# Reordering the prelude of an mLSTM-and-two-gated-layers kernel: exponents, reciprocals, first weights and gate columns

## The reference

```
m_new  = max(f + m, i);  f_stab = exp(f + m - m_new);  i_stab = exp(i - m_new)
C = f_stab*C + i_stab * v k^T;   n = f_stab*n + i_stab*k
y = sigmoid(o) * (C q) / max(|n q|, 1)
```

```
x1  = silu(rmsnorm(y) @ w_gate) * (rmsnorm(y) @ w_val) @ w_out       (d_ff = 1536)
out = sigmoid(x1 @ w_gate2) * (x1 @ w_val2) @ w_out2
```

## Time and profile before

| | |
|---|---|
| times of the runs | 470.47, 470.62, 474.57 us; median 470.62 us |
| profiled execution | 470.63 us, span 468.8 us |
| mean granted TensorE clock | 0.999 |
| TensorE matmul busy | 457.6 us, 98% |
| VectorE busy | 225.5 us, 48% |
| ScalarE busy | 184.9 us, 39% |
| GpSimd busy | 27.0 us, 6% |

### The profile page before, as it was taken

How to read it: one execution, slowest core, us unless ns; L and a number is a source line. 1 busy time by engine, 2 the same in 40 slices (tenths; PEclk the granted TensorE clock), 3 DMA queues, 4 the chain that set the end, 5 groups by cost and what they waited for, 6 DMA issues and landing times.

```text
span 468.8 us, 7881 instructions
## 1 busy us (share of the span) xinstructions
PE 457.6 (98%) x3064; PEld 377.5 (81%) x3064; DVE 225.5 (48%) x447; ACT 184.9 (39%) x379; POOL 27.0 (6%) x59
## 2 busy tenths in 40 slices
PE   7899899999999999999999999999999999999997
PEld 4588888878888887888888888888888888888885
DVE  5988657776566453645455552222322222322222
ACT  6755545543543432454454552222322222322222
POOL 4311101101010000000000000000000000000000
PEclk9999999999999999999999999999999999999999
DMA  7664035630201300002322200000000000100001
GB/s 211 193 208 127 24 98 174 197 91 15 72 22 38 124 2 0 2 0 95 97 96 95 83 0 0 2 0 1 25 31 1 0 1 0 57 1 0 1 0 57
DMA packets 15757, 26.30 MB, mean 56 GB/s; under 512 B 2248, under 2 KB 10664, under 8 KB 15720
## 3 DMA queue, kind: packets, MB, share of 16 engines
q1 hardware_dynamic: 15496, 25.68, 17.9%
q10 hardware_dynamic: 224, 0.12, 0.1%
HBM read 23.55 MB, written 1.97 MB: 54 GB/s over the span
## 4 chain that ended last, share of the span: by engine, by line
PE 85%; issue 6%; DVE 5%; ACT 1%; POOL 1%; DMA 1%; SPq 0%; DVEq 0%; POOLq 0%; ACTq 0%
PE bank L1346 50%; PE bank L1408 7%; PE bank L1409 6%; PE bank L1410 6%; PE bank L1416 3%; PE bank L1417 3%; PE pair L1286 2%; PE pair L1263 1%; PE bank L1353 1%; PE pair L1300 1%; PE pair L1252 1%; PE bank L1318 1%; DVE gv_split L1012 1%; PE bank L1333 1%; DMA fi_row<-fi_first 1%
## 5 line engine op out<-in xcount | busy, mean ns | idle before, releaser
L1346 PE MATMUL bank<-x_hi,gv_split 128*128 128x512 f32 (+1 forms) x780 | 236.8, 374 | 2.3 <-DVE hid L1028 1.8
L1346 PEld LDWEIGHTS bank<-x_hi,gv_split 128*128 128x128 f32 x780 | 143.1, 188 | 29.1 <-issue 3.3
L1346 PE MATMUL bank<-x_lo,gv_split 128*128 128x512 f32 (+1 forms) x436 | 161.4, 373 | 0.0
L1041 DVE TENSOR_TENSOR hid<-hid,bank 128x512 f32<-128x512 f32 x48 | 33.0, 687 | 132.4 <-PE bank L1346 132.4
L611 ACT ACTIVATE hid_hi<-hid 128x512 fp32r<-128x512 f32 (+1 forms) x78 | 46.6, 598 | 121.4 <-DVE hid L1041 90.5
L1346 PEld LDWEIGHTS bank<-x_lo,gv_split 128*128 128x128 f32 x436 | 82.0, 188 | 14.2
L604 ACT ACTIVATE hid<-bank 128x512 f32<-128x512 f32 (+1 forms) x78 | 43.9, 562 | 118.0 <-PE bank L1346 87.3
L1048 DVE TENSOR_TENSOR hid_lo<-hid,hid_hi 128x512 fp32r<-128x512 f32 (+1 forms) x78 | 51.3, 658 | 42.7 <-ACT hid_hi L611 42.7
L1408 PE MATMUL bank<-hid_hi,wo_split 128*128 128x512 f32 (+1 forms) x154 | 59.7, 388 | 0.0
L1410 PE MATMUL bank<-hid_hi,wo_split 128*128 128x512 f32 (+1 forms) x154 | 57.5, 373 | 0.0
L1409 PE MATMUL bank<-hid_lo,wo_split 128*128 128x512 f32 (+1 forms) x154 | 57.5, 373 | 0.0
(11 more groups left out here) (164 smaller groups left out, 354.9 us busy)
## 6 DMA issues: line engine op xcount, KB each, us to landing
gv_raw<-wgv SPq DMA_DIRECT2D x24, 384.0 KB, 3.1
qk_tile<-qk SPq DMA_DIRECT2D x24, 160.0 KB
wo_raw<-wo SPq DMA_DIRECT2D x24, 160.0 KB, 3.2
v_sb<-v SPq DMA_DIRECT2D x12, 168.0 KB, 4.3
gate<-og SPq DMA_DIRECT2D x12, 160.0 KB, 3.7
k_sb<-k SPq DMA_DIRECT2D x10, 160.0 KB, 4.5
outT<-y_out SPq DMA_DIRECT2D x6, 256.0 KB, 2.0
outT<-y_tail SPq DMA_DIRECT2D x3, 128.0 KB, 2.3
```

The lines of the kernel that those rows point to most:

```text
L1041: ins = nc.vector.tensor_tensor(h, h, v_ps[:, 0:size], ALU.mult)
L1346: mm = pe.matmul(ps[:, 0:size], lhs, rhs, start=(i == 0), stop=whole and i == len(passes) - 1)
```

## The change

All of it lies in the prelude and unit 0.

- TensorE issues all four `early_exponents` ahead of the four `early_outputs`. GpSimd makes the four copies that these need (`select_rows`) ahead of `keep_logs(1)`; copies 2 and 3 wait for exponents 2 and 3.
- The denominators of tiles 0 and 1 lie in one tile and get one `max` and one reciprocal (`first_denominators`), which wait for both `magnitude`s. `first_quotients(0)`, `first_quotients(1)` and `apply_gate(1)` follow.
- The rest of the first weights is made in two halves: the gate half in front of `weight_rows(0)`, the value half behind `rest_x(1)`. `round_gv(0)` on ScalarE moves ahead of `raise_gate` and of both `magnitude`s, `gate_tanh(1)` ahead of `magnitude(0)`.
- `load_gv(0)` is issued ahead of the two `load_gate`.
- `turn_gates(0)` leaves the prelude; it, `turn_gates(1)` and `exponents(2)` now follow `value_products(0)` instead of standing around `gate_products(0)`.

```diff
+            load_gv(0)
             load_gate(0)
             load_gate(1)
-            load_gv(0)
...
-            for i in range(2):
+            for i in range(4):
                 select_rows(i)
             keep_logs(1)
-            for i in range(2, 4):
-                select_rows(i)
...
             gate_tanh(0)
+            round_gv(0)
             raise_gate()
+            gate_tanh(1)
             magnitude(0)
-            gate_tanh(1)
-            round_gv(0)
             magnitude(1)
...
+            def first_denominators():
+
+                dve.wait_ge(abs_done, B)
+                nc.vector.tensor_scalar(den_first[1][:], den_first[0][:], 2.0, None, ALU.max).then_inc(den_done, 2 * B)
+                dve.wait_ge(den_done, 2 * B)
+                nc.vector.reciprocal(den_first[2][:], den_first[1][:]).then_inc(rden_done, B)
...
+            def rest_first(which):
+                dve.wait_ge(gv_rounded, 1)
+                nc.vector.tensor_tensor(wgv[0][:, which, 3:6], gv_raw[0][:, which], wgv[0][:, which, 0:3].bitcast(F32),
+                                        ALU.subtract).then_inc((gate_ready, gv_ready)[which], 1)
...
             early_weigh(3)
+            rest_first(0)
             weight_rows(0)
-            normalise(0)
-            normalise(1)
+            first_denominators()
+            first_quotients(0)
+            first_quotients(1)
+            apply_gate(1)
             sum_logs(1)
             less_log(1)
             early_scale(0)
             rest_logs(1)
             early_scale(1)
-            rest_gv(0)
             rest_x(0)
             rest_x(1)
+            rest_first(1)
             weight_rows(1)
...
             scores(1)
+            early_exponents(2)
+            early_exponents(3)
             early_outputs(0)
             keep_clock_up(WARM[8], True)
-            early_exponents(2)
+            early_outputs(1)
             keep_clock_up(WARM[9], True)
-            early_exponents(3)
-            early_outputs(1)
             keep_clock_up(WARM[3])
...
             turn_x(1)
-            turn_gates(0)
             keep_clock_up(WARM[7])
...
                 gate_products(u)
-                if u == 0:
-                    turn_gates(1)
-                    exponents(SCORE_AT[u])
                 if early:
                     turn_x(TURN_AT[u])
                 if u == 1:
                     state_sums(1)
                 value_products(u)
+                if u == 0:
+                    turn_gates(0)
+                    turn_gates(1)
+                    exponents(SCORE_AT[u])
```

More of the change, by code:

```diff
@@ L192, in build @@
             den, rden = sba("den", [P, H]), sba("rden", [P, H])
-            den_abs = [sba(f"den_abs{t}", [P, H]) for t in range(B)]
+            den_first = [sba(f"den_first{i}", [P, B, H]) for i in range(3)]
             y1, y1_first = sba("y1", [P, H, D]), sba("y1_first", [P, H, D])
@@ L259, in build @@
             sem(n) for n in ("gv_rounded", "gv_ready", "wo_rounded", "wo_ready"))
-        yhi_done, swap_done, tail_done, y_moved, out0_ready, out1_ready, out1_last, tail_part = (
-            sem(n) for n in ("yhi_done", "swap_done", "tail_done", "y_moved", "out0_ready", "out1_ready", "out1_last", "tail_part"))
+        yhi_done, swap_done, tail_done, y_moved, out0_ready, out1_ready, out1_last, tail_part, gate_ready = (
+            sem(n) for n in ("yhi_done", "swap_done", "tail_done", "y_moved", "out0_ready", "out1_ready", "out1_last", "tail_part", "gate_ready"))
         block = ctx.enter_context(nc.Block())
@@ L541, in magnitude @@
                 out = pv_ps(2 * t)[:, 0:H * DV].rearrange("p (h d) -> p h d", h=H)
-                nc.scalar.activation(den_abs[t][:], out[:, :, D], ACT.Abs, scale=2.0).then_inc(abs_done, 1)
+                nc.scalar.activation(den_first[0][:, t], out[:, :, D], ACT.Abs, scale=2.0).then_inc(abs_done, 1)
             def gate_tanh(t):
@@ L958, in normalise @@
             def normalise(t):
[L960 to L965, removed]
-                need(dve, rden_done, t)
[L967 to L974, removed]
+                dve.wait_ge(comb_done, t - B + 1)
+                out = hsum[:].rearrange("p g h d -> p (g h) d")
+                need(dve, rden_done, t)
+                nc.vector.tensor_scalar(den[:], out[:, :, D], -2.0, 2.0, ALU.mult, ALU.max).then_inc(den_done, 1)
+                dve.wait_ge(den_done, 2 * t + 1)
+                nc.vector.scalar_tensor_tensor(out=den[:], in0=out[:, :, D], scalar=2.0, in1=den[:],
+                                               op0=ALU.mult, op1=ALU.max).then_inc(den_done, 1)
                 dve.wait_ge(den_done, 2 * t + 2)
@@ L978, in normalise, with first_quotients, apply_gate @@
                 dve.wait_ge(rden_done, t + 1)
-                if t > 1:
-                    dve.wait_ge(y_done, t - 1)
+                dve.wait_ge(y_done, t - 1)
                 nc.vector.tensor_tensor(y1_of(t)[:], out[:, :, 0:D], rden[:].unsqueeze(2).broadcast_to([P, H, D]),
                                         ALU.mult).then_inc(y1_done, 1)
-                if t == 0:
-                    return
+                apply_gate(t)
+            def first_denominators():
[3 more added lines that the diff above has]
+                nc.vector.reciprocal(den_first[2][:], den_first[1][:]).then_inc(rden_done, B)
+            def first_quotients(t):
+                dve.wait_ge(rden_done, B)
+                dve.wait_ge(att_out, 2 * t + 2)
+                out = pv_ps(2 * t)[:, 0:H * DV].rearrange("p (h d) -> p h d", h=H)
+                nc.vector.tensor_tensor(y1_of(t)[:], out[:, :, 0:D],
+                                        den_first[2][:, t].unsqueeze(2).broadcast_to([P, H, D]), ALU.mult).then_inc(y1_done, 1)
+            def apply_gate(t):
                 dve.wait_ge(y1_done, t + 1)
@@ L1357, in gate_products @@
                 part, b, f, start, size = UNIT_LIST[u]
-                if part == 0 and b == 0:
+                if u == 0:
+                    pe.wait_ge(gate_ready, 1)
+                elif part == 0 and b == 0:
                     pe.wait_ge(gv_ready, f + 1)
@@ L1378, in value_products @@
                 need(pe, hid_done, u)
+                if u == 0:
+                    pe.wait_ge(gv_ready, 1)
                 mm = hidden(v_ps, 1, f, start, size, not has_group(u))
```

## The result

The changed kernel takes **476.71 us** (median of four executions: 473.37, 476.57, 476.85, 476.87), the kernel before 470.57. The ratio is 1.009, with a 95% interval of 1.0052 to 1.0128. I had forecast 472.1 us and a range up to 473.9: the loss is there, but it is four times as large as the forecast +1.45 us. The profiled execution is one of 476.85 us, its span 475.0 (before 468.8), its mean granted clock 0.985 (before 0.999).

The account below looks back on a forecast made before the run. TensorE, busy nearly the whole span, was taken as the bound, with VectorE's chain passing delays on. A later unit 0 start (+0.4) and delay within it (+1.05) gave +1.45 us on 470.63, 472.1 us; range 470.0 to 473.9.

Parts of the forecast that it names:

- X, the start of unit 0: End of the prelude: unit 0's start goes from 20.96 to about 21.35, +0.4 us; bounds -0.25 and +0.8.
- the landing worked out from the price per KB: Prelude loads: at 3.3 ns per KB, weights land at 11.3 and gate tile 0 at 11.8, so `gate_tanh(0)` starts at 11.9.
- the price of `round_gv(0)` and `gate_tanh(1)` ahead of `magnitude(0)`: ScalarE's prelude list: the first denominator starts near 14.27 instead of 13.22, 1.05 us later on tile 0.
- the 0.4 allowed: Prelude, tile 1's gating: ends at 15.80, or up to 0.4 us later where it overlaps GpSimd.
- Unit 0: Within unit 0: VectorE weighs tile 2 at 6.4 us after unit 0's start against 5.36, +1.05; bounds +0.5 and +1.9.
- VectorE's wait at `take_columns(0)`: Unit 0: VectorE stands idle 1.4 us until `turn_gates(0)`, now behind the value products, is done.
- `c_diag`: Unit 0, VectorE: starting before `vw`, it takes 0.2 us instead of 0.68, which is the upper bound.
- The sum without the clock: Whole kernel: +0.4 for unit 0's start and +1.05 within unit 0 make +1.45 us, 472.1 us; chance 0.70.
- The clock: Rival: in the prelude's 2.0 us gap before the first transpose TensorE's clock falls, adding 1.3 to 2.5 us: 474.0; chance 0.08.
- Not slower: Rival: unit 0 starts 0.25 us earlier and its loss goes into a later 1.6 us wait: 470.3 or 469.6; chance 0.20.

Follow-up runs that it names:

- columns and exponents: Kernel before with `turn_gates` and `exponents(2)` moved behind `value_products(0)` and with `early_exponents` first, nothing else: median 473.33 us, ratio 1.0046.
- changed, swap: Changed kernel with `result_products(9)` ahead of `state_sums(4)` in unit 10: median 471.71 us, ratio 1.0028.
- results first: Kernel before with `result_products(9)` ahead of `state_sums(4)` in unit 10: median 470.20 us, ratio 0.997.
- first columns back: Changed kernel with `turn_gates(0)` back in the prelude; `turn_gates(1)` and `exponents(2)` stay behind `value_products(0)`: median 472.46 us, ratio 1.0011.
- fillers in unit 0: Changed kernel with five filler matmuls in unit 0, two behind `turn_gates(0)` and three behind `exponents(2)`: median 473.06 us, ratio 1.0017.
- exponents back: Changed kernel with the exponents and GpSimd's copies in their old order: median 474.43 us, ratio 1.0073.
- loads back: Changed kernel with the two gate tiles loaded ahead of the first weights again: median 473.98 us, ratio 1.0067.
- changed, again: The changed kernel run once more, nothing altered, for more executions: median 475.82 us, ratio 1.009 to the kernel before.
- fillers in the prelude: Changed kernel with 21 instead of 14 fillers ahead of the first transpose: median 476.87 us, ratio 1.0092.
- third group: Follow-up runs on one chip meant to take TensorE's holes away; the kernel before, run beside them, had median 472.31 us.
- changed, fillers in unit 0, swap: Changed kernel with five filler matmuls in unit 0 and `result_products(9)` ahead of `state_sums(4)` in unit 10: median 471.29 us, ratio 0.9994.

## Why the prediction was wrong

**X, the start of unit 0.** Forecast +0.4, measured +0.14 in the profile. The tanh did wait for its tile, as worked out, but until 11.53 and not 11.90; the second profile has 12.00, and the mean of the eight profiles with this order of loads and exponents is 11.5. So the landing worked out from the price per KB came about 0.4 us too late. Everything behind it (rounding, two magnitudes, one denominator, GpSimd's gating, the mean squares) took its old distances, and `apply_gate(1)` took 0.85 us beside GpSimd, within the 0.4 allowed. The sentence on the price of `round_gv(0)` and `gate_tanh(1)` ahead of `magnitude(0)`, 1.05 us, was the one to build on: "columns and exponents", without that price, starts unit 0 at 19.77.

**Unit 0.** Forecast +1.05, measured +1.06. VectorE's wait at `take_columns(0)` was 1.50 us for my 1.4, `c_diag` 0.15 for my 0.2, the exponential began 4.00 us behind X for my 4.0. `vw(0)` and `rest_gv(1)` did meet, `vw` taking 1.47 us for 0.75, and `scores(2)` started at X+5.17 of my 5.1 to 5.25. In "changed, swap", where no clock has to be taken out, VectorE weighs at X+6.41 for my 6.4.

**The sum without the clock.** Forecast +1.45. The cleanest measurement is the changed kernel with fillers and swap against "results first", both without falls: 471.21 against 470.20, +1.0 us, from two groups run apart; without fillers 471.09, +0.9. In the profiles of "results first" and "changed, swap" the first products of unit 5 start 1.37 us apart (47.93 and 49.30), close to the forecast. The wait for `vw` near 72 us is then 0.3 us shorter in the second (0.32 for 0.62); whether that is loss swallowed or the load's variation one profile each can't tell. The mechanism was right and the size within half a microsecond.

**The clock** is the step that failed: a term that the sum put at nothing and that measured 5 us in the changed kernel. I wrote "If the granted clock fell in the new gap and stayed low for 2.5 to 5 us, 1.3 to 2.5 us would be added: 474.0", and gave it 0.08. Three things in it were wrong. The place: I looked only at the largest new hole, 2.0 us in the prelude, and not at unit 0, where the new order has three small holes among small matmuls; closing the prelude's hole left 5 long falls in 6. The length: the low stretch was 13.7 us and cost 5 us; 2.5 us was taken from the start-up fillers, where TensorE has nothing but full-size work. The chance: "the granted clock reads 1.00 through the existing gap" took one execution as proof, when one of the three times in front of me, 474.57, lay 4 us off the others. Of the 111 later executions of the kernel before 8 lost as much clock as that time suggests, and another 51 have a short fall. Why three holes of 0.2 to 0.4 us bring the clock down, in about half of the executions, stays open.

**"Not slower"** was wrong as argued: the later wait for VectorE, 1.6 us, is still 1.6 to 1.7 us in every kernel that has no fillers there, and swallowed nothing.

**`c_diag`.** Ahead of `vw` it took 0.15 us; in "first columns back", where it again starts 0.1 behind `vw`, 0.68. This bears out what the prediction took from the Trainium skill ("SBUF — State Buffer", section "Who interferes with whom"): of such a pair of instructions the one that is issued first holds up the other.

## What to carry to other kernels

Before moving work on TensorE, lay out its new timeline and look for stretches in which short waits and small matmuls come together, not only for the longest wait; here three waits of 0.2 to 0.4 us cost 5 us, when they cost anything. Test the parts of a change apart: one of these was worth 1.2 us at the start of unit 0, and the others hid it. Where the times of one kernel fall into steps, read the mean clock of each execution and compare those without a fall first: the step between the groups is the clock's price, the rest is the order's. And try other work in a hole: `result_products` ahead of `state_sums` was worth 2.1 us of median in its group, for a reordering worth 0.3 by itself.

## What the hardware showed that I had not expected

- The low stretches came in three lengths: 3.4 us ("fillers in unit 0", "exponents back", "columns and exponents", "loads back"; mean clock 0.995 or 0.996), 6.8 us ("changed, again"; 0.992) and 13.7 us (the changed kernel and "fillers in the prelude"; 0.985). They cost about 2.3 us (kernel before in the third group, 472.9 for 470.5), 3 to 4 us and 5 us (changed kernel with the swap: none 471.1, 473.9 and 474.9 at 0.993, 475.9 to 476.4 at 0.985).
- In the three profiles with a long fall it begins at 26.9, 27.0 and 26.8 us, while `scores(2)` starts at 26.27, 26.09 and 26.76. So the fall doesn't follow that instruction.
- The moment at which the clock is raised at the start differs between executions of nearly the same program. It can be read from the 12 start-up fillers, which last from 4.12 to 5.30 us in these profiles, here in the changed kernel:

```profile
1.31 5.27 PE L1233 MATMUL bank<-fill 128*128 128x512 bf16 x12 [1.31 <-POOL keep_log L401]
```

  Whether the later fall depends on that moment stays open: the three profiles with a fall near 26.9 us have the long fillers (5.22 to 5.30 us), but "columns and exponents" (5.30), "first columns back" (5.28) and "changed, fillers in unit 0, swap" (5.30) have them too and don't fall there.
- The hole of 1.6 us ahead of unit 5 caused no fall in the 12 executions of "results first", while the hole of 1.04 us at 70 us seems to have caused most of the short ones of the kernel before. I can't say from these runs what makes the difference: the swap shortened that hole and changed the matmuls around it at once, and no experiment did one without the other.
